# A convolution and SwiGLU kernel: a new order of work for its first three tiles

## Chip, cores and metric

One core of one Trainium2 chip. The metric is device time in microseconds (us), the median of several executions.

## The reference

`x` is [4, 4096, 192], `weight_gen` [4, 4096, 8, 7], `w_gate` and `w_val` [192, 1536], `w_out` [1536, 192].

```python
w = softmax(weight_gen, axis=-1)                # 7 taps per token and head
out = einsum('bshk,bskhg->bshg', w, x_unf)      # causal convolution: token s and the 6 before it
xn = out / sqrt(mean(out * out) + 1e-6) * rms_g
g, val = xn @ w_gate, xn @ w_val
return (silu(g) * val) @ w_out
```

## The kernel before

Each of the 128 partitions holds 128 neighbouring tokens. A tile is four tokens of each partition (`J` = 4, `N` = 512 tokens), so there are 32 tiles, `T` = 0 to 31. Every engine runs its own list of instructions; semaphores written by hand order them.

For a tile, VectorE normalizes the taps (4 steps, `norm_step`) and convolves (13 steps, `conv_step`: 7 products, 6 additions), 17 steps in all. ScalarE squares (`square`), GpSimd makes the inverse root (`inverse_rms`), ScalarE scales (`scale`), TensorE transposes (`turn_x`). ScalarE writes the high part of the transposed tile (`x_high`), VectorE the low part (`x_low`). The up projections have K = 192 as three slots of 64 rows, and gate and value use the two halves of the array side by side; slots 1 and 2 want halves of `xT` on the other partitions, which three DMAs bring (`copy_halves`).

TensorE then makes 12 blocks `f` of 128 hidden columns: `hidden(T, t, f)` is 18 matmuls (w_hi x_hi, w_lo x_hi, w_hi x_lo for three slots and gate and value). ScalarE takes silu, VectorE multiplies (`h`), ScalarE rounds (`h_hi`), VectorE subtracts (`h_lo`), and `project` adds two blocks into `out_ps` with 32 matmuls. `turn_after(T)` is the block after which the next tile is turned: `xf`. `up_ps` has two pairs of banks, so a `hidden` waits for the silu and the product of the block two before it. `out_low` (ScalarE) and `out_add` (VectorE) empty `out_ps` before the next tile's first `project`.

VectorE weaves the 17 steps of tile T + 2 among the blocks of tile T by the list `steps_other`. The first tiles have lists of their own. Tile 0's convolution is made ahead of everything, three tokens of four by VectorE and one by GpSimd; tile 1's by GpSimd alone while tile 0 is multiplied. SyncE issues every DMA. The taps of tiles 3 to 31 get their maxima, differences and exponentials in three pieces (5, 12 and 12 tiles) during tiles 0, 1 and 2; between an exponential and a silu ScalarE loads a function table. TensorE makes 84 transposes of the identity that nobody reads (L699) in the middle of tile 0's convolution.

Of the kernel before, what the change touches and what calls it, by code (L numbers as in the profile page):

```python
# [5 lines left out]
ALU = mybir.AluOpType  # L6
# [7 lines left out]
P = 128  # L14


def dynconv_swiglu(nc, x, weight_gen, w_gate, w_val, w_out, rms_g, out):
# [21 lines left out]
    FIRST = 3  # L39
# [12 lines left out]
    with ExitStack() as ctx:  # L52
# [25 lines left out]
        tap_w1 = sb("tap_w1", [P, J * H, K])  # L78
# [3 lines left out]
        prod_pool = sb("prod_pool", [P, J * D])  # L82
# [31 lines left out]
        x_zeroed = sem("x_zeroed")  # L114
        pool_zeroed = sem("pool_zeroed")
# [19 lines left out]
        x_lo_done = sem("x_lo_done")  # L135
        x_copied = sem("x_copied")
# [25 lines left out]

        cuts = [FIRST, 8, 20, TILES]
        pieces = [slice(a * J * H, b * J * H) for a, b in zip(cuts, cuts[1:])]
# [42 lines left out]
        J0 = J - 1  # L207
        WARM_TURNS = 84
        NORM0_DONE, FIRST_DONE, NORM1_DONE = NORM, MIX, MIX + NORM

        @block.sync
        def _(sp):
# [5 lines left out]

            sp.dma_start(x_first[16:P, 0:PAD, :], x_d[15:P - 1, TOK - PAD:TOK, :]).then_inc(halo_loaded, 16)
            sp.dma_start(x_first[1:16, 0:PAD, :], x_d[0:15, TOK - PAD:TOK, :]).then_inc(halo_loaded, 16)  # L220
            load_taps(0)
            for n in range(2):
                sp.dma_start(x_first[:, PAD + n * J:PAD + (n + 1) * J, :],
                             x_d[:, n * J:(n + 1) * J, :]).then_inc(xfirst_loaded[n], 16)
                if n == 0:
                    load_taps(1)
            sp.dma_start(gains[:, 0:1], g_d[0:P, :]).then_inc(gains_loaded, 16)
            for s in (1, 2):
                for m in range(2):
                    c = CHUNKS[m][s]  # L230
                    sp.dma_start(gains[m * DB:(m + 1) * DB, s:s + 1], g_d[c * DB:(c + 1) * DB, :]).then_inc(gains_loaded, 16)
            for s in range(SLOTS):
                for m, w in enumerate((w_gate, w_val)):
                    c = CHUNKS[m][s]
                    sp.dma_start(raw[m * DB:(m + 1) * DB, s, :], w[c * DB:(c + 1) * DB, :]).then_inc(w_loaded[s], 16)
# [23 lines left out]
            def turn(i, loads=True, first=False, last=False):  # L259
                for t in range(2):  # L260
                    T = 2 * i + t
                    if not (first and t == 0):
                        store(T - 1, (t + 1) % 2)
                    if not (last and t == 1):
# [15 lines left out]
        def _(pool):  # L280
            nc.gpsimd.memset(ident[:], 0.0).then_inc(pool_steps, 1)
            nc.gpsimd.memset(minus_half[:], -0.5).then_inc(pool_steps, 1)
            nc.gpsimd.memset(eps_rms[:], EPS_RMS).then_inc(pool_steps, 1)
            nc.gpsimd.memset(zero[:], 0.0).then_inc(pool_steps, 1)
            pool.wait_ge(pool_steps, 4)
            nc.gpsimd.affine_select(out=ident[:], in_=ident[:], compare_op=ALU.not_equal, fill=1.0, base=0,
                                    pattern=[[-1, P]], channel_multiplier=1).then_inc(consts_done, 1)
# [45 lines left out]
        def _(act):  # L333
# [395 lines left out]
```

## Time and profile before

| | us |
|---|---|
| median of 3 runs | 1323.94 (1322.46 to 1326.7) |
| the profiled execution | 1322.03 |
| its span, first to last instruction | 1320.2 |
| TensorE busy in the span | 1277.4 |
| mean granted TensorE clock | 0.992 |

Times in the trace count from the start of the span; 1.83 us of the profiled execution lie around it. Busy shares are means over the start, the first tiles and the steady tiles, which are read apart below.

### The profile page before, as it was taken

Reading aid. Unit: us, or ns where it says so; the run is one execution under the profiler, and the core shown is the slowest. Engines: PE = TensorE matmul, PEld = TensorE weight load, DVE = VectorE, ACT = ScalarE, POOL = GpSimd, SP = SyncE. Lnnn points to the kernel's source line nnn. Section 1 sums busy time; section 2 is a strip of 40 time slices with the busy share of each in tenths; the row PEclk is TensorE's granted clock in tenths of the full one; section 3 lists DMA queues with packets and bytes.
Section 4 is the critical chain, followed back from the end, with each engine's and each line's share of the span. In section 5 each row is a group of like instructions: output and inputs, shape, how many; then the busy total and the mean of one; then the engine's idle time right before and its main releaser. Section 6 shows DMA issues by size and latency. Waiting matters only on the chain.

```text
span 1320.2 us, 33644 instructions
## 1 busy us (share of the span) xinstructions
PE 1277.4 (97%) x13524; PEld 1260.1 (95%) x13524; DVE 992.0 (75%) x1441; ACT 662.8 (50%) x1427; POOL 83.3 (6%) x101
## 2 busy tenths in 40 slices
PE   3798999999999999999999999999999999999998
PEld 3687889999999999999999999999999999999998
DVE  6788877777777778777778777777777777777653
ACT  4364565445555445555444555444555444555543
POOL 7600000000000000000000000000000000000000
PEclk9799999999999999999999999999999999999999
DMA  9121211211221211221211221111121121121010
GB/s 307 38 67 27 65 58 52 67 56 37 67 67 43 67 55 37 67 67 43 67 55 41 63 67 48 62 55 56 47 67 60 50 67 55 37 67 37 14 37 13
DMA packets 20101, 77.69 MB, mean 59 GB/s; under 512 B 3215, under 2 KB 5007, under 8 KB 19854
## 3 DMA queue, kind: packets, MB, share of 16 engines
q1 hardware_dynamic: 19982, 75.83, 18.9%
q8 instruction: 108, 1.77, 0.5%
q14 instruction: 11, 0.09, 0.0%
HBM read 38.07 MB, written 12.58 MB: 38 GB/s over the span
## 4 chain that ended last, share of the span: by engine, by line
PE 89%; DVE 5%; issue 2%; ACT 2%; DMA 1%; POOL 0%; SPq 0%; POOLq 0%
PE up_ps L620 59%; PE out_ps L651 26%; PE out_ps L655 3%; DVE y L203 1%; DVE h L544 1%; DVE h_lo L562 1%; DMA xT<-xT 1%; DVE prod L201 1%; PE up_ps L588 1%; ACT taps L391 0%; ACT silu L410 0%; PE up_ps L592 0%; DMA taps<-in_weight_gen 0%; ACT h_hi L417 0%; DVE y L201 0%
## 5 line engine op out<-in xcount | busy, mean ns | idle before, releaser
L620 PE MATMUL up_ps<-xT,w_hi 64*128 64x512 f32 x4608 | 858.1, 396 | 14.9 <-DMA xT<-xT 6.5
L620 PEld LDWEIGHTS up_ps<-xT,w_hi 64*128 64x128 f32 x4608 | 627.3, 186 | 26.1 <-issue 8.1
L620 PE MATMUL up_ps<-xT,w_lo 64*128 64x512 f32 x2304 | 589.2, 395 | 0.0
L651 PE MATMUL out_ps<-wo,h_hi 64*128 64x384 f32 x3072 | 478.2, 354 | 3.1 <-issue 2.7
L655 PE MATMUL out_ps<-wo,h_lo 64*128 64x192 f32 x3072 | 453.3, 247 | 0.0
L544 DVE TENSOR_TENSOR h<-up_ps,silu 128x512 f32<-128x512 f32 x384 | 264.7, 689 | 234.1 <-ACT silu L410 233.8
L651 PEld LDWEIGHTS out_ps<-wo,h_hi 64*128 64x128 f32 x3072 | 425.8, 185 | 5.1 <-issue 3.9
L655 PEld LDWEIGHTS out_ps<-wo,h_lo 64*128 64x128 f32 x3072 | 421.2, 187 | 0.5
L417 ACT ACTIVATE h_hi<-h 128x512 fp32r<-128x512 f32 x384 | 242.7, 632 | 352.3 <-DVE h L544 292.0
L410 ACT ACTIVATE silu<-up_ps 128x512 f32<-128x512 f32 x384 | 228.7, 595 | 263.7 <-PE up_ps L620 259.5
L620 PEld LDWEIGHTS up_ps<-xT,w_lo 64*128 64x128 f32 x2304 | 349.5, 187 | 3.3
L562 DVE TENSOR_TENSOR h_lo<-h,h_hi 128x512 fp32r<-128x512 f32 x384 | 265.2, 691 | 40.2 <-ACT h_hi L417 40.2
L203 DVE TENSOR_TENSOR y<-y,prod 128x768 f32<-128x768 f32 (+1 forms) x186 | 177.4, 954 | 2.1
L201 DVE TENSOR_TENSOR prod<-x_buf,tap_w 128x768 f32<-128x768 f32 x180 | 171.1, 951 | 1.5
L292 POOL TENSOR_TENSOR mean_sq<-sq_mean,eps_rms 128x4 f32<-128x4 f32 x32 | 8.2, 258 | 1149.2 <-ACT xn L367 1149.2
L374 ACT ACTIVATE xn<-y,inv_rms 128x128 f32<-128x128 f32 (+1 forms) x256 | 74.1, 360 | 4.4 <-POOL inv_rms L294 4.4
L525 DVE TENSOR_TENSOR last<-out_ps,last 128x768 f32<-128x768 f32 x32 | 30.6, 957 | 27.4 <-ACT last L397 27.4
L367 ACT ACTIVATE xn<-y 128x192 f32<-128x192 f32 x128 | 44.4, 348 | 1.6 <-DVE y L203 1.6
L294 POOL TENSOR_TENSOR inv_rms<-mean_sq,minus_half 128x4 f32<-128x4 f32 x32 | 34.0, 1064 | 2.5
L470 DVE TENSOR_TENSOR xT<-up_ps,xT 128x512 fp32r<-128x512 f32 x32 | 22.1, 691 | 10.7 <-ACT xT L381 9.2
L201 DVE TENSOR_TENSOR y<-x_buf,tap_w 128x768 f32<-128x768 f32 x30 | 28.7, 957 | 1.0
L473 DVE TENSOR_TENSOR xT<-up_ps,xT 64x256 fp32r<-64x256 f32 x64 | 26.6, 416 | 1.0
(43 smaller groups left out, 311.4 us busy)
## 6 DMA issues: line engine op xcount, KB each, us to landing
x_buf<-in_x SPq DMA_DIRECT2D x30, 960.0 KB, 4.5
xT<-xT SPq DMA_DIRECT2D x96, 256.0 KB, 3.8
result<-last SPq DMA_DIRECT2D x32, 384.0 KB, 2.3
taps<-in_weight_gen SPq DMA_DIRECT2D x1, 3248.0 KB, 19.5
raw<-in_moe_w_gate SPq DMA_DIRECT2D x3, 384.0 KB, 6.3
raw<-in_moe_w_val SPq DMA_DIRECT2D x3, 384.0 KB, 7.3
last<-in_moe_w_out SPq DMA_DIRECT2D x1, 1152.0 KB, 12.4
x_first<-in_x SPq DMA_DIRECT2D x2, 384.0 KB, 4.6
```

Source lines behind the costliest of these rows:

```text
L201: return engine.tensor_tensor(heads(product if n else acc), heads(flat(src[:, k + j0:k + j1, :])), w[:, q0:q1, k].unsqueeze(2).to_broadcas ...
L203: return engine.tensor_tensor(acc, acc, product, ALU.add)
L294: nc.gpsimd.tensor_tensor(inv_rms[:], mean_sq[:], minus_half[:], ALU.pow).then_inc(rms_done, 1)
L367: nc.scalar.activation(xn[:, j * D:(j + 1) * D], y[:, t, j, :], ACT.Square, scale=D ** -0.5, accum_out=sq_mean[:, j:j + 1]).then_inc(squar ...
L374: nc.scalar.activation(part[:, j, :], y[:, t, j, d], ACT.Copy, scale=inv_rms[:, j:j + 1]).then_inc(xn_done, 1)
L410: nc.scalar.activation(silu[:, f % 2, :], gate_ps[:, b, :], ACT.Silu).then_inc(silu_done, 1)
L417: nc.scalar.activation(h_hi[:, f % HB, :], h[:, f % 2, :], ACT.Copy).then_inc(h_hi_done, 1)
L544: nc.vector.tensor_tensor(h[:, f % 2, :], val_ps[:, b, :], silu[:, f % 2, :], ALU.mult).then_inc(h_done, 1)
L562: nc.vector.tensor_tensor(h_lo[:, f % HB, :], h[:, f % 2, :], h_hi[:, f % HB, :].bitcast(F32), ALU.subtract).then_inc(h_lo_done, 1)
L620: mm = nc.tensor.matmul(ps[:, banks, :], w[rows, s, cols], xT[rows, t, s, part, :], start=(s == 0 and n == 0), stop=ends)
L651: nc.tensor.matmul(out_ps[:, j, 0:2 * D], h_hi[rows, g % HB, cols], wo[rows, g, :, :].rearrange("p a d -> p (a d)"), start=(g == 0 and k < ...
L655: mm = nc.tensor.matmul(out_ps[:, j, 0:D], h_lo[rows, g % HB, cols], wo[rows, g, 0, :], start=False, stop=(g == FB - 1 and k >= 2), skip_g ...
```

## The change

Start-up: SyncE loads tile 0's taps first; ScalarE issues the gains and the three `w_val` pieces, SyncE the `w_gate` pieces. GpSimd convolves nothing any more. VectorE makes tile 0's seven products over all four tokens into seven tiles, adds the last two, and TensorE sums the six that result with float32 matmuls by the identity (`sum_first`, L704) in `out_ps`, from where they are squared and scaled (half by VectorE, `scale_rest`). There are 50 idle transposes from the start on and 30 after the sum.

Tiles 0 and 1: copies by ScalarE and VectorE inside the engines take the place of `copy_halves` (`x_high_moved`, `x_low_moved`), and the first `hidden` of each takes the matmuls with x_lo last. `w_lo` and `wo` are made in halves. Tile 1 is convolved by VectorE during tile 0, and is squared, scaled and turned only when tile 0's last `project` is through.

From tile 1 on: the lookahead grows from one tile to two by `steps_early`; `turn_after` goes 11, 9, 7, 5. The taps of tiles 4 to 7 are prepared in tile 1, those of later tiles one by one (two in each tile 3 to 14), and their exponentials are taken in tiles 2, 5, 9 and 15. The tile loops of ScalarE and VectorE are written out.

```diff
-    FIRST = 3
+    FIRST = 4
-            return 9 if isinstance(T, int) and T == 0 else 5
+            return {0: 11, 1: 9, 2: 7}.get(T, 5) if isinstance(T, int) else 5
+        exps_at = {(2, 1): (FIRST, 8), (5, 9): (8, 12), (9, 9): (12, 20), (15, 9): (20, TILES)}
-        WARM_TURNS = 84
+        WARM_TURNS, KEEP_TURNS = 50, 30
@@ sync
+            load_taps(0)
 ...
-            load_taps(0)
...
+            load_first(0)
+            load_w(0)
+            load_w(1)
+            load_taps(1)
+            load_w(2)
+            load_first(1)
...
-            copy_halves(0, 0)
@@ scalar
+            first_exps(0)
+            for s in range(SLOTS):
+                act.dma_start(raw[DB:P, s, :], w_val[c * DB:(c + 1) * DB, :]).then_inc(w_loaded[s], 16)
+            w_high(0)
+            w_high(1)
             square(0, 0, range(J))
-            scale(0, 0, range(J))
-            x_high(0, 0, 1)
+            w_high(2)
+            scale(0, 0, range(J // 2))
+            first_exps(1)
+            x_high_moved(0, 0, 1)
@@ scalar, tile
-                squares_at, scales_at = (xf - 4, xf - 3) if first else (0, 1), (xf - 2, xf - 1) if first else (2, 3)
+                squares_at, scales_at = {9: ((6,), (7,)), 7: ((4,), (5, 6)), 5: ((0, 1), (2, 3))}.get(xf, ((), ()))
@@ vector
+            def x_low_moved(T, t, banks):
+                dve.wait_ge(x_hi_done, 3 * T + 1)
+                for to, of in moves(t, 0)[0:2]:
+                    nc.vector.tensor_copy(to, of).then_inc(mid_hi_moved, 1)
+...
+                to, of = moves(t, 1)[2]
+                nc.vector.tensor_copy(to, of).then_inc(end_lo_moved, 1)
-            steps_first = [0, 0, 2, 2, 0, 2, 2, 2, 2, 2, 2, 1]
-            steps_taps = [2, 2, 2, 0, 2, 2, 2, 0, 2, 1, 1, 1]
+            seconds = [0, 0, 1, 1, 2, 2, 2, 1, 2, 2, 0, 0]
+            steps_early = [(2, 4), (2, 2), (2, 2), (2, 2), (2, 2), (2, 2), (2, 3), (3, 0), (3, 0), (3, 0), (3, 4), (3, 2),
...
@@ tensor
+            def sum_first():
+                for k in range(K - 1):
+                    pe.wait_ge(first_mix, NORM + k + 1 if k < K - 2 else FIRST_DONE)
+                    for b in range(2):
+                        cols = slice(b * 2 * D, (b + 1) * 2 * D)
                        mm = nc.tensor.matmul(out_ps[:, b, 0:2 * D], ident[:], first_prods[k][:, cols],
                                              start=(k == 0), stop=(k == K - 2))
...
+                if first:
+                    project(T, FB - 2)
+                    pe.wait_ge(silu_done, xf)
+                    pe.wait_ge(h_done, xf)
+                    pe.wait_ge(xn_done, 4 * J)
+                    turn_x(1, 1, pair(0, xf + 1))
```

TensorE's list at the start. Before:

```order
L699 MATMUL up_ps<-ident 128x128 x84
L588 MATMUL up_ps<-ident,xn 128x64 x8
L592 MATMUL up_ps<-ident,xn 128x64 x4
L620 MATMUL up_ps<-xT,w_hi 128x512 x2
L620 MATMUL up_ps<-xT,w_lo 128x512 x2
L620 MATMUL up_ps<-xT,w_hi 128x512 x4
```

The same place after the change; L862 and L865 are the idle transposes, L715 and L720 the turn, L766 the first `hidden`:

```order
L862 MATMUL up_ps<-ident 128x128 x50
L704 MATMUL out_ps<-prod,ident 128x384 x2
L704 MATMUL out_ps<-y,ident 128x384 x4
L704 MATMUL out_ps<-xn,ident 128x384 x2
L704 MATMUL out_ps<-prod_first,ident 128x384 x2
L704 MATMUL out_ps<-h,ident 128x384 x2
L865 MATMUL up_ps<-ident 128x128 x30
L715 MATMUL up_ps<-ident,xn 128x64 x8
L720 MATMUL out_ps<-ident,xn 128x64 x4
L766 MATMUL up_ps<-xT,w_hi 128x512 x2
```

Twelve matmuls of 384 columns came in, and the idle transposes stand on both sides of them.

VectorE's list from the end of tile 0's tap norm. Before, the first three of 13 steps over 576 columns, each waiting for the one ahead:

```order
L190 TENSOR_TENSOR tap_w<-taps,tap_inv 128x224 [waits first_mix]
L447 TENSOR_REDUCE tap_max<-taps 128x64 [waits first_loaded1,first_mix]
L449 TENSOR_TENSOR taps<-taps,tap_max 128x448 [waits first_steps]
L201 TENSOR_TENSOR y<-x_first,tap_w 128x576 [waits pool_zeroed,x_zeroed,xfirst_loaded0]
L201 TENSOR_TENSOR prod<-x_first,tap_w 128x576 [waits first_mix]
L203 TENSOR_TENSOR y<-y,prod 128x576 [waits first_mix]
```

After the change, in the same place:

```order
L212 TENSOR_TENSOR tap_w<-taps,tap_inv 128x224 [waits first_mix]
L575 TENSOR_TENSOR prod<-x_first,tap_w 128x768 [waits halo_zeroed,halo_loaded,last_zeroed,xfirst_loaded0,first_mix]
L575 TENSOR_TENSOR y<-x_first,tap_w 128x768 x2
L575 TENSOR_TENSOR xn<-x_first,tap_w 128x768
L575 TENSOR_TENSOR prod_first<-x_first,tap_w 128x768
L575 TENSOR_TENSOR h<-x_first,tap_w 128x768
L575 TENSOR_TENSOR silu<-x_first,tap_w 128x768
L578 TENSOR_TENSOR h<-h,silu 128x768 [waits first_mix]
L556 SCALAR_TENSOR_TENSOR w_lo<-raw,gains,w_hi 128x768 [waits w_hi_done] x2
L495 TENSOR_REDUCE tap_max<-taps 128x96 [waits first_loaded1]
```

Thirteen steps became eight, and the other taps' maxima moved behind them.

ScalarE's list in tile 2, where the first late exponential stands (L445 is `out_low`, L458 the silu):

```order
L439 ACT_TABLE_LOAD
L439 ACTIVATE taps<-taps 128x896 [waits rest_less]
L445 ACTIVATE last<-out_ps 128x768 [waits bank_left]
L458 ACT_TABLE_LOAD [waits h_done]
L458 ACTIVATE silu<-up_ps 128x512 [waits gate_done]
```

Before, no exponential stood ahead of an `out_low`; those of the three pieces stood behind block 9.

## Rows read from the trace of the kernel before

**Rows 1.** The page: busy time, share and instructions of each engine.
```profile
PE 1277.4 (97%) x13524; PEld 1260.1 (95%) x13524; DVE 992.0 (75%) x1441; ACT 662.8 (50%) x1427; POOL 83.3 (6%) x101
```

**Rows 2.** Windows: us, busy time and count of each engine, clock, DMA.
```profile
0.00:32.70 32.70, 11.82 (x96) 11.43 (x96) 21.30 (x27) 13.58 (x26) 23.01 (x29) 0.95 0.96 310
32.70:90.70 58.00, 48.26 (x456) 42.54 (x458) 44.33 (x57) 29.04 (x58) 24.02 (x13) 0.88 0.19 53
90.70:212.80 122.10, 114.88 (x1195) 104.44 (x1193) 97.95 (x132) 65.85 (x130) 3.62 (x6) 0.99 0.16 47
212.80:1310.00 1097.20, 1097.20 (x11719) 1096.90 (x11718) 825.35 (x1223) 552.07 (x1212) 32.60 (x54) 1.00 0.18 53
```

**Rows 3.** Timeline: block starts of TensorE, tile 1, then tile 4.
```profile
90.72 0.42 PE L620 MATMUL up_ps<-xT,w_hi 64*128 64x512 f32 x2
...
212.87 0.45 PE L620 MATMUL up_ps<-xT,w_hi 64*128 64x512 f32 x2
...
217.08 0.38 PE L651 MATMUL out_ps<-wo,h_hi 64*128 64x384 f32 x2
...
219.34 0.45 PE L620 MATMUL up_ps<-xT,w_hi 64*128 64x512 f32 x2
```

**Rows 4.** Timeline of the start, all engines: start, duration, instruction, idle before.
```profile
0.74 0.42 SPq L219 DMA_DIRECT2D x_first<-in_x  x1
...
1.73 0.36 SPq L215 DMA_DIRECT2D taps<-in_weight_gen  x1
...
6.61 2.34 ACT L346 ACTIVATE x_first<-zero 1x1152 f32<-1x1152 f32 x2
...
8.19 0.62 DVE L447 TENSOR_REDUCE tap_max<-taps 128x64 f32<-128x448 f32 x1
...
9.39 1.08 DVE L201 TENSOR_TENSOR y<-x_first,tap_w 128x576 f32<-128x576 f32 x1
...
15.73 10.92 PE L699 MATMUL up_ps<-ident 128*128 128x128 f32 x84 [15.73 <-DVE prod L201]
...
19.25 1.58 ACT L352 ACTIVATE w_hi<-raw,gains 128x1536 fp32r<-128x1536 f32 x1 [1.84 <-DMA raw<-in_moe_w_val]
...
22.89 0.36 ACT L367 ACTIVATE xn<-y 128x192 f32<-128x192 f32 x1 [1.60 <-DVE y L203]
...
24.46 1.76 POOL L292 TENSOR_TENSOR mean_sq<-sq_mean,eps_rms 128x4 f32<-128x4 f32 x1 [2.22 <-ACT xn L367]
26.30 2.47 POOL L294 TENSOR_TENSOR inv_rms<-mean_sq,minus_half 128x4 f32<-128x4 f32 x1
```

**Rows 5.** Timeline from the first turn on, all engines.
```profile
31.09 0.69 PE L588 MATMUL up_ps<-ident,xn 64*128 64x64 f32 x8 [4.44 <-ACT xn L374]
...
34.90 1.81 SPq L251 DMA_DIRECT2D xT<-xT  x3
...
40.48 0.80 PE L620 MATMUL up_ps<-xT,w_hi 64*128 64x512 f32 x2 [5.61 <-DMA xT<-xT]
...
43.44 0.60 ACT L410 ACTIVATE silu<-up_ps 128x512 f32<-128x512 f32 x1 [6.82 <-PE up_ps L620]
```

**Rows 6.** Windows of the early drop of the clock; columns as in rows 2.
```profile
29.20:40.40 11.20, 2.92 (x18) 1.54 (x18) 3.68 (x4) 6.38 (x13) 10.73 (x7) 0.50 0.73 256
40.50:46.20 5.70, 5.70 (x28) 4.48 (x30) 2.13 (x2) 1.23 (x2) 5.46 (x4) 0.50 0.01 3
```

**Rows 7.** Groups by line and form: count, busy us, mean ns, idle before.
```profile
L544 DVE TENSOR_TENSOR h<-up_ps,silu 128x512 f32<-128x512 f32 x384 | 264.7, 689 | 234.1 <-ACT silu L410 233.8
...
L203 DVE TENSOR_TENSOR y<-y,prod 128x768 f32<-128x768 f32 x180 | 171.2, 951 | 1.9
...
L473 DVE TENSOR_TENSOR xT<-up_ps,xT 64x256 fp32r<-64x256 f32 x64 | 26.6, 416 | 1.0
...
L391 ACT ACTIVATE taps<-taps 128x2688 f32<-128x2688 f32 x2 | 4.9, 2452 | 0.0
...
L294 POOL TENSOR_TENSOR inv_rms<-mean_sq,minus_half 128x4 f32<-128x4 f32 x32 | 34.0, 1064 | 2.5
```

More of the change, by code:

```diff
@@ L263, in turn @@
                         store(T - 1, (t + 1) % 2)
-                    if not (last and t == 1):
+                    if not (first and t == 0 or last and t == 1):
                         copy_halves(T + 1, 1 - t)
@@ L410, in tile @@
                     nc.scalar.activation(silu[:, f % 2, :], gate_ps[:, b, :], ACT.Silu).then_inc(silu_done, 1)
-                    if f == xf and not last:
+                    if first and f in (0, 4):
+                        wo_high(f // 4)
+                    if f == xf and not (first or last):
                         x_high(T + 1, 1 - t, pair(t, xf + 1))
@@ L609, in hidden @@
                 cols = slice(f * P, (f + 1) * P)
-                for s in range(SLOTS):
-                    if f == 0 and s == 1:
-                        pe.wait_ge(x_copied, 48 * (T + 1))
-                    for n, (w, part) in enumerate(((w_hi, 0), (w_lo, 0), (w_hi, 1))):
-                        if isinstance(T, int) and T == 0 and f == 0:
-                            first_wait(s, n)
-                        ends = s == SLOTS - 1 and n == 2
-                        for m, (ps, done) in enumerate(((gate_ps, gate_done), (val_ps, val_done))):
-                            rows = slice(m * DB, (m + 1) * DB)
-                            mm = nc.tensor.matmul(ps[:, banks, :], w[rows, s, cols], xT[rows, t, s, part, :],
-                                                  start=(s == 0 and n == 0), stop=ends)
-                            if ends:
-                                mm.then_inc(done, 1)
+                parts = ((w_hi, 0), (w_lo, 0), (w_hi, 1))
@@ new lines, in hidden @@
+                steps = [(s, n) for s in range(SLOTS) for n in range(3)]
+                if T < 2 and f == 0:
+                    steps.sort(key=lambda at: at[1] == 2)
+                for at, (s, n) in enumerate(steps):
+                    w, part = parts[n]
+                    if T < 2 and f == 0:
+                        first_wait(T, s, n)
+                    elif f == 0 and s == 1 and n == 0:
+                        pe.wait_ge(x_copied, 48 * (T - 1))
+                    ends = at == len(steps) - 1
+                    for m, (ps, done) in enumerate(((gate_ps, gate_done), (val_ps, val_done))):
+                        rows = slice(m * DB, (m + 1) * DB)
+                        mm = nc.tensor.matmul(ps[:, banks, :], w[rows, s, cols], xT[rows, t, s, part, :],
+                                              start=(at == 0), stop=ends)
+                        if ends:
+                            mm.then_inc(done, 1)
@@ L676, in tile @@
                     if f == 0:
-                        if not first:
+                        if T > 1:
                             project(T - 1, FB - 2)
```

407 lines of the change are left out of this document (256 added, 151 removed).

## The prediction

> **What bounds the kernel now.** I read the page first: TensorE is busy for 97% of the span and VectorE for 75% [rows 1]. That is a mean, so the windows come next. From 212.8 us to 1310 us TensorE is busy in every microsecond, at full clock [rows 2]. A faster VectorE, ScalarE or DMA is worth nothing there, and the change leaves TensorE's work there as it is. All it can win or lose lies ahead of 212.8 us, in three stages: 32.7 us in which TensorE does no useful work, 58 us with 48 busy at a clock of 0.88, and 122 us with 115 busy.
>
> The price of work without waits comes from the block starts of tile 4 [rows 3]: two `hidden` take 217.08 - 212.87 = 4.21 us (2.1 each), two blocks' `project` 2.26, so 6.47 a pair of blocks. Six pairs and a turn (12 transposes, 0.69 us at half clock [rows 5], so some 0.4) make 39.2 us a tile. I measure progress at two marks [rows 3]: A, when tile 0 is projected and tile 1's first two `hidden` are done (90.72), and B, the start of tile 4 (212.87). Between them lie three tiles less one pair, 3 x 39.2 - 6.5 = 111.1 us of work in 122.15, so 11 us are waits.
>
> **The change, part by part.** *To the first sum.* The taps' DMA is issued at 0.74 instead of 1.73, so the tap norm, which ended at 8.19 [rows 4], ends near 7.2. The next maxima (8.19 to 9.39) move out of the way. But the products wait for the zeroing of the halo. ScalarE now issues three DMAs first (an issue is 0.42 on SyncE [rows 4]; I take 0.5 to 0.6) and then zeroes one row, half of 2.34: 6.61 - 1.0 + 1.7 + 1.2 = 8.5. So VectorE stands from 7.2 to 8.5. Seven products and one addition at 0.95 [rows 7] are 7.6 us: 16.1. No row shows a float32 matmul of 384 columns. The nearest row is 84 transposes of the same matrix in 10.92 us [rows 4], 0.13 us per 128 columns, so 0.39. From below the pair of 384 columns within `project` (2.26 us for 16 pairs of 384 or 192 columns, at most 0.2), from above twice the row, 0.78. I take 0.39, whose row has the same operand: a pair, 0.78, hides behind a product of 0.95 and only the last pair shows. Squares start at 16.8 instead of 22.89.
>
> The Trainium skill has a rule against this. *FP8 and Floating Point Precision*, TensorE Precision Notes, says that true float32 takes four passes through the array. By it, 4 x 384 columns at 2.4 GHz are 0.64 us a matmul (an estimate from the page), a pair no longer hides behind its product, and the squares start some 0.6 us later; no row of this trace shows it.
>
> *Sum to turn.* It takes 31.09 - 22.89 = 8.2 us now. GpSimd's two small steps take 1.76 + 2.47 [rows 4] where the power alone is 1.06 on the mean [rows 7]: VectorE was making `w_lo` beside it. VectorE still makes two halves of `w_lo` and the maxima there, so I take 1.9 for the two steps, from 1.4 alone to 4.2. Squares 1.6, scaling halved to 1.2 since VectorE does half. The turn comes at 21.5: 16.8 + 1.6 + 1.9 + 1.2. `w_high(2)` (1.58) stands between squares and scaling, beside GpSimd. It waits for the last weights, whose conversion began at 19.25 [rows 4]; it is free at 18.4 now.
>
> If the two queues work side by side the weights come earlier. The Trainium skill speaks against that: *SBUF — State Buffer*, "Can I just issue two DMAs to hit both halves?", says that two such DMAs serialize on the same 16 engines. By it the third piece would land about as before and the turn move by up to 0.8 us; the row's DMA wait agrees that the weights were late, but shows one queue only.
>
> *Turn to first silu.* Now 43.44 - 31.09 = 12.35 us, 5.6 of them from the DMA issue at 34.90 to 40.48 [rows 5]. The DMA goes. In its place: the exponential of the early taps 0.7, `x_high` main 0.6 (the first row at 22.8), two copies of 64x512 by VectorE, its subtractions 0.69 + 2 x 0.42 [rows 7], the last copy; on ScalarE two rests, one copy, then two after the low part. A copy of 64x512 has no row; 0.42 is the nearest from below (half as long, [rows 7]), 0.69 from above; I take 0.6. The chain is 22.8, 24.0 (copies), 24.7, 25.5, 26.1, plus three pairs of matmuls: gate at 26.5. ScalarE is through at 25.9 and loads the silu table until 27.2. First silu at 27.2, **16.2 us earlier**.
>
> *Tile 0 and mark A.* After that silu 11 `hidden` of tile 0, two of tile 1, six `project` and a turn are 41.3 us of work; now they take 47.3. VectorE's list in tile 0 is 24 products and differences at 0.6 to 0.69, 13 conv steps at 0.95, and three half `w_lo` and two half `wo` (by their length at the conv rate 5 to 6): 34 us beside 38 us of TensorE, with GpSimd's convolution gone from beside it. So tile 0 flows. But tile 1 is no longer turned under cover. The last gate comes at 26.5 + 11 x 2.1 + 4 x 2.26 = 58.6; silu, product, `h_hi` and `h_lo` at 0.6 to 0.69 each, with ScalarE and VectorE just busy, make 61.9, and the last `project` ends at 64.2. ScalarE's squares end at 62.8, rms 64.2, scaling 65.4, turn 65.8, and the chain of copies as above (4.3 us) gives the first gate at 70.1. So TensorE stands for most of 64.2 to 70.1, in which 2.5 us of matmuls fit: a new stall of 3.5. Mark A falls at 72.2 instead of 90.72, **18.5 earlier**.
>
> *Tiles 1 to 3.* The 11 us of waits between A and B do not go; they change place. VectorE has 23 conv and norm steps in tile 1, 26 in tile 2 (22 of them convolutions, 21 us), 19 in tile 3. With 14.5 for 24 block steps (0.69 each alone [rows 7], some 0.6 back to back), 1.5 for `x_low` and 1 for `out_add`, tile 2 holds 39.5 us for a tile of 39.2: VectorE has no slack. Places: tile 1's first `project` waits for `out_add` because four `hidden` follow one another (1.1); in block 6 of tile 1 and 4 of tile 2 ScalarE's squares wait for three conv steps, and the next silu behind them. From the gate on: silu and product 1.3, conv 2.9, squares 1.6, silu and product 1.3, so 7.1, where the second `hidden` after it wants them after 2.1 + 2.26 + 2.1 = 6.5; with VectorE late by 0.6 and 1.2 that is 1.2 and 1.8; the turns wait for the eight scalings just ahead (31.09 less 28.77, 2.3 [rows 4, 5]), 1.5 and 2.4; `rest_subtract` ahead of a product (0.9); tile 2's exponential with two table loads ahead of `out_low` (1). Sum 9.9, and 0.5 of small ones: 10.4 against 11. **0.6 earlier.** The shift of later exponentials, up to 12 tiles' worth (2.45 us [rows 7], and two table loads), falls into steady tiles; only the longest, in tile 15, may overrun the two pairs of banks, **0.5 later**.
>
> *The clock.* Now it is at half, 1.2 GHz, from 29.2 to 46.2 [rows 6]: it fell after the warm transposes ended at 26.65 and rose after work without gap from 40.48. Only the 5.7 busy us from 40.5 cost, 2.9 us. After the change TensorE stands twice: 22 to 26.5, in pieces, and 64 to 70. I expect the clock to fall after either. A return took 5.7 us of full work at half clock, so each costs 0 to 2.9; I take 2 for the second and 1.5 for the first: **3.5 later**.
>
> *Sum*: 16.2 earlier at the silu grows to 18.5 at A, 19.1 at B; less 0.5 and 3.5 it is 15.1, say 15 us. The profiled span of 1320.2 becomes 1305, its execution 1307 (1.8 more). The median of the runs before, 1323.94, is 1.9 above the profiled one; I predict the median: 1323.94 - 15 = **1309 us**.
>
> **Rivals.** *The clock holds and the weave is smooth.* Idle transposes bridge the first gap, the conv steps end before the squares are asked for. Speaks for it: tiles 1 to 3 get a turn later than before, when more is ready. Against: VectorE's 39.5 us in tile 2. It gives back 3.5 and some 3 of the 10.4: 1300 to 1305. Chance 0.17.
>
> *The start is slower than reckoned, or VectorE falls behind.* The upper ends: sums at 0.78 (1.5), GpSimd blocked (2.3), weights late (0.8), clock at its upper bound twice (2.3), stalls in tiles 1 and 2 half as long again (5). Some of these together, 5 to 10 us: 1313 to 1319. For it: each stall above starts from VectorE having no slack. Chance 0.18.
>
> *No change.* The waits only move: TensorE stands as long in tiles 1 and 2 as it gained. It needs 15 us of new waits on top of the 10.4, with VectorE's load at most 39.5 a tile; 1320 to 1328. Chance 0.05.
>
> *Slower.* The tile loops of VectorE and ScalarE are now straight code that must be fetched. A fetch that comes late stalls a silu or a product. VectorE is idle for a quarter of a steady tile [rows 2], 9.7 us; beyond that cover a late fetch shows. It decides at 15 us over 28 steady tiles, 0.54 us of visible stall a tile; at 1 us a tile the time is 1337. Against it: TensorE's 13524 matmuls [rows 1] are straight code already and show no gap after 212.8. Chance 0.05.
>
> **Numbers.** My forecast has 0.55, with its own range 1305 to 1313. The range of 1302 to 1316 leaves out the faster end of the first rival, the far end of the second, and the last two: 2 in 10. Faster by over 0.3% (about what a measurement of this kernel can tell from no change) 0.90, within it 0.05, slower 0.05.
>
> **What would show it.** Right: squares near 17, turn near 21.5, first silu near 27, marks A and B near 74 and 197, TensorE without a gap afterwards, two drops of the clock, near 25 and 67. Wrong: the sum's matmuls over 0.7 us each; GpSimd's power over 2 us; the first product later than 9; gaps of TensorE after mark B; a third stretch at half clock.

## The result, and the profile after

The changed kernel takes 1299.21 us (median of 4 runs, 1298.18 to 1300.5) where the kernel before took 1323.2 (1322.24 to 1326.7, now four runs): a ratio of 0.9816 with an interval of 0.9801 to 0.9831, 24 us faster where 15 were forecast, and outside the range. The profiled execution took 1299.58 with a span of 1297.4, so the spans differ by 22.8. Line numbers have moved in the changed kernel: L766 is `hidden`, L806 and L810 `project`, L715 and L720 the turn, L704 the sum, L649 `h`, L458 the silu.

The page of the changed kernel, its busy times (compare [rows 1]) and its row of the clock over the slices: TensorE does as much, 4 us less of busy time, and its clock shows no slice below 9 tenths.

```profile
PE 1273.1 (98%) x13544; PEld 1240.3 (96%) x13544; DVE 1001.0 (77%) x1511; ACT 663.9 (51%) x1428; POOL 42.8 (3%) x76
...
PEclk9999999999999999999999999999999999999999
```

The windows up to the first `hidden`, up to mark A, up to mark B and behind it; columns as in [rows 2]. The first stage is 9 us shorter, the clock is 1.00 in every stage, and behind B there are 3.4 us without TensorE where there were none.

```profile
0.00:23.70 23.70, 19.65 (x116) 15.84 (x117) 14.77 (x24) 11.12 (x21) 5.12 (x14) 1.00 0.92 246
23.70:73.10 49.40, 45.42 (x458) 40.54 (x460) 41.10 (x66) 26.48 (x52) 1.21 (x2) 1.00 0.23 97
73.10:195.00 121.90, 113.42 (x1196) 103.07 (x1193) 105.06 (x154) 60.65 (x133) 3.96 (x6) 1.00 0.19 55
195.00:1293.00 1098.00, 1094.62 (x11784) 1080.81 (x11780) 839.07 (x1269) 564.99 (x1224) 32.53 (x54) 1.00 0.18 53
```

The timeline of the start, all engines (compare [rows 4]). The first product comes at 8.89; the sum's matmuls of one product fill 1.3 us (13.88, 15.17, 16.46; a float32 matmul leaves two records, so x4 is a pair); squares at 18.13, the turn at 22.33, the first silu at 27.82.

```profile
8.89 0.96 DVE L575 TENSOR_TENSOR prod<-x_first,tap_w 128x768 f32<-128x768 f32 x1 [2.07 <-DMA x_first<-in_x]
...
13.88 1.45 PE L704 MATMUL out_ps<-xn,ident 128*128 128x384 f32 x4
...
15.17 1.45 PE L704 MATMUL out_ps<-prod_first,ident 128*128 128x384 f32 x4
...
16.46 1.45 PE L704 MATMUL out_ps<-h,ident 128*128 128x384 f32 x4
...
18.13 0.31 ACT L392 ACTIVATE xn<-out_ps 128x192 f32<-128x192 f32 x1
...
19.55 0.20 POOL L328 TENSOR_TENSOR mean_sq<-sq_mean,eps_rms 128x4 f32<-128x4 f32 x1 [11.03 <-ACT xn L392]
19.78 1.58 ACT L372 ACTIVATE w_hi<-raw,gains 128x1536 fp32r<-128x1536 f32 x1 [0.32 <-DMA raw<-in_moe_w_val]
19.82 1.02 POOL L330 TENSOR_TENSOR inv_rms<-mean_sq,minus_half 128x4 f32<-128x4 f32 x1
...
22.33 0.46 PE L715 MATMUL up_ps<-ident,xn 64*128 64x64 f32 x8 [1.14 <-ACT xn L400]
...
23.59 0.88 DVE L528 CAST xT<-xT 64x512 fp32r<-64x512 f32 x2 [0.79 <-ACT xT L412]
...
27.82 0.60 ACT L458 ACTIVATE silu<-up_ps 128x512 f32<-128x512 f32 x1
```

TensorE's block starts in tile 4 (compare [rows 3]), then the starts of tiles 17 and 28.

```profile
194.95 0.44 PE L766 MATMUL up_ps<-xT,w_hi 64*128 64x512 f32 x2
...
199.10 0.36 PE L806 MATMUL out_ps<-wo,h_hi 64*128 64x384 f32 x2
...
201.38 0.44 PE L766 MATMUL up_ps<-xT,w_hi 64*128 64x512 f32 x2
...
705.47 0.48 PE L766 MATMUL up_ps<-xT,w_hi 64*128 64x512 f32 x2
...
1134.07 0.47 PE L766 MATMUL up_ps<-xT,w_hi 64*128 64x512 f32 x2
```

The same starts of tiles 17 and 28 in the kernel before:

```profile
723.50 0.41 PE L620 MATMUL up_ps<-xT,w_hi 64*128 64x512 f32 x1
...
1155.61 0.41 PE L620 MATMUL up_ps<-xT,w_hi 64*128 64x512 f32 x1
```

These are eleven tiles with no wait in either. From start to start, one took before the change (1155.61 - 723.50) / 11 = 39.28 us; now (1134.07 - 705.47) / 11 = 38.96. The instructions are the same. The `hidden` pair shows it (199.10 - 194.95 = 4.15, where [rows 3] have 4.21) and `project` does not (2.28 against 2.26).

So the gain of the span is: first silu 15.6 earlier (43.44 to 27.82); mark A 17.7 (90.72 to 73.06); mark B 17.9 (212.87 to 194.95); behind B, 28 tiles of 0.32 less make 8.9, and new waits in tiles 6 to 16 take back 4.0. 17.9 + 8.9 - 4.0 = 22.8. (The profiled executions differ by 22.45, because 2.2 us instead of 1.8 lie around the span. The medians differ by 24.0: that of before lies 1.2 above its profiled execution, that of the changed kernel 0.4 below.) The prediction had no term for the 8.9.

### The profile page after: what moved, and what is told of

It reads as the page before. It is cut to its first block, busy times and chain, and to the rows that moved or that the text cites. A ratio compares the mean times of both kernels' runs of the same rounds, so it can differ in the third digit from the quotient of the medians.

```text
span 1297.4 us, 32473 instructions
## 1 busy us (share of the span) xinstructions
PE 1273.1 (98%) x13544; PEld 1240.3 (96%) x13544; DVE 1001.0 (77%) x1511; ACT 663.9 (51%) x1428; POOL 42.8 (3%) x76
## 4 chain that ended last, share of the span: by engine, by line
PE 86%; DVE 6%; ACT 3%; issue 3%; DMA 1%; ACTq 0%; POOL 0%; DVEq 0%
PE up_ps L766 55%; PE out_ps L806 21%; PE out_ps L810 9%; DVE h L649 2%; DVE y L225 1%; DMA raw<-in_moe_w_val 1%; DVE prod L223 1%; DVE h_lo L675 1%; ACT silu L458 1%; PE up_ps L715 1%; ACT L458 0%; ACT xn L400 0%; ACT L439 0%; ACT xn L392 0%; PE up_ps L720 0%
## 5 line engine op out<-in xcount | busy, mean ns | idle before, releaser
L766 PE MATMUL up_ps<-xT,w_hi 64*128 64x512 f32 x4608 | 816.2, 392 | 8.5 <-DVE h L649 5.4
L766 PEld LDWEIGHTS up_ps<-xT,w_hi 64*128 64x128 f32 x4608 | 527.2, 184 | 25.9 <-issue 8.6
L766 PE MATMUL up_ps<-xT,w_lo 64*128 64x512 f32 x2304 | 502.5, 387 | 0.0
L806 PE MATMUL out_ps<-wo,h_hi 64*128 64x384 f32 x3072 | 465.0, 356 | 7.1 <-issue 2.4
L810 PE MATMUL out_ps<-wo,h_lo 64*128 64x192 f32 x3072 | 437.2, 247 | 0.0
L649 DVE TENSOR_TENSOR h<-up_ps,silu 128x512 f32<-128x512 f32 x384 | 264.6, 689 | 209.0 <-ACT silu L458 205.9
L806 PEld LDWEIGHTS out_ps<-wo,h_hi 64*128 64x128 f32 x3072 | 357.5, 184 | 11.2 <-issue 3.3
L810 PEld LDWEIGHTS out_ps<-wo,h_lo 64*128 64x128 f32 x3072 | 362.4, 187 | 0.9
L458 ACT ACTIVATE silu<-up_ps 128x512 f32<-128x512 f32 x384 | 227.9, 594 | 246.0 <-PE up_ps L766 237.5
L766 PEld LDWEIGHTS up_ps<-xT,w_lo 64*128 64x128 f32 x2304 | 269.2, 185 | 6.3
L225 DVE TENSOR_TENSOR y<-y,prod 128x768 f32<-128x768 f32 x186 | 177.3, 953 | 2.1
L400 ACT ACTIVATE xn<-y,inv_rms 128x128 f32<-128x128 f32 x244 | 70.6, 360 | 1.4 <-POOL inv_rms L330 1.4
L445 ACT ACTIVATE last<-out_ps 128x768 f32<-128x768 f32 x32 | 25.3, 790 | 3.7 <-PE out_ps L810 3.7
## 6 DMA issues: line engine op xcount, KB each, us to landing
last<-in_moe_w_out SPq DMA_DIRECT2D x1, 1152.0 KB, 18.1
x_first<-in_x SPq DMA_DIRECT2D x2, 384.0 KB, 10.8
```

The lines of the kernel that those rows point to most:

```text
L225: return engine.tensor_tensor(acc, acc, product, ALU.add)
L400: nc.scalar.activation(part[:, j, :], src, ACT.Copy, scale=inv_rms[:, j:j + 1]).then_inc(xn_done, 1)
L458: nc.scalar.activation(silu[:, f % 2, :], gate_ps[:, b, :], ACT.Silu).then_inc(silu_done, 1)
L649: nc.vector.tensor_tensor(h[:, f % 2, :], val_ps[:, b, :], silu[:, f % 2, :], ALU.mult).then_inc(h_done, 1)
L766: mm = nc.tensor.matmul(ps[:, banks, :], w[rows, s, cols], xT[rows, t, s, part, :], start=(at == 0), stop=ends)
L806: nc.tensor.matmul(out_ps[:, j, 0:2 * D], h_hi[rows, g % HB, cols], wo[rows, g, :, :].rearrange("p a d -> p (a d)"), start=(g == 0 and k < ...
```

## The experiments

**Where do 0.32 us a tile come from?** The change also removes the tile `tap_w1` (224 floats, 896 bytes of each partition), in which GpSimd kept tile 1's taps, so everything declared behind it, `xT` among it, lies 896 bytes lower. Theory A: the addresses set the pitch of the `hidden` matmuls, the time from one start to the next. Its rival: the new order of work does. `x1_pad` gives the changed kernel a tile that nobody uses and that puts `xT` where it was; `x2_shift` gives the kernel before the new addresses.

```diff
# x1_pad, on the changed kernel
         tap_w = sb("tap_w", [P, J * H, K])
+        spare = sb("spare", [P, J * H, K])
# x2_shift, on the kernel before: the declaration moves to the end
-        tap_w1 = sb("tap_w1", [P, J * H, K])
...
+        tap_w1 = sb("tap_w1", [P, J * H, K])
```

> The changed kernel with one unused tensor of 896 bytes a partition put back where the removed tap_w1 stood, so that every tensor declared behind it has the address it had before the change. A steady tile takes 38.96 us in the changed kernel and 39.28 us in the one before, though TensorE has the same list there. Theory A (where xT, w and h lie in SBUF sets the pitch of the matmul pairs): a steady tile returns to 39.28 us and the time rises by 27 x 0.32 = 8 to 9 us, to about 1308 us. Theory B (the pitch comes from something else in the change, such as the written-out loops or the clock): a steady tile stays at 38.96 and the time at about 1299 us.

> The kernel before with tap_w1 declared last, so that the tensors behind it move down by 896 bytes a partition; nothing else changes. Theory A: a steady tile takes 38.96 us instead of 39.28 and the time falls by 9 to 10 us, to about 1314 us. Theory B: no change, 1323 us.

`x1_pad` took 1308.76 (1307.33 to 1310.02), a ratio to before of 0.9894 (0.9877 to 0.991): the new order of work alone is worth 13.8 us against the 1322.55 of the same chip. (Its four executions are 1307.33, 1307.5 and twice 1310.02, with a mean granted clock of 1.000, 1.000 and twice 0.996, so the 13.8 is good to some 1.3 us.) `x2_shift` took 1314.75 (1314.71 to 1315.21), 0.9937 (0.9921 to 0.9954): the kernel before gains 7.8 us from a declaration that moves. Starts of tiles 17 and 28 of `x1_pad`:

```profile
709.00 0.45 PE L767 MATMUL up_ps<-xT,w_hi 64*128 64x512 f32 x2
...
1141.08 0.45 PE L767 MATMUL up_ps<-xT,w_hi 64*128 64x512 f32 x2
```

And of `x2_shift`:

```profile
720.84 0.46 PE L620 MATMUL up_ps<-xT,w_hi 64*128 64x512 f32 x2
...
1149.44 0.45 PE L620 MATMUL up_ps<-xT,w_hi 64*128 64x512 f32 x2
```

(1141.08 - 709.00) / 11 = 39.28 us a tile in the changed kernel, (1149.44 - 720.84) / 11 = 38.96 in the kernel before: the tile goes with the addresses in both. The order of work as the cause fell; theory A stands. `x1_pad` starts tile 4 at 194.70, so ahead of mark B the addresses gained nothing. `x2_shift` gained less than 28 x 0.32 = 9 us: its profiled execution reaches mark B 1.45 us later than before (214.32 against 212.87), with one more drop of the clock in tile 0.

**Do the idle transposes keep the clock up?** `x3_nokeep` takes away the 30 behind the sum.

```diff
-        WARM_TURNS, KEEP_TURNS = 50, 30
+        WARM_TURNS, KEEP_TURNS = 50, 0
```

> The changed kernel without the 30 idle transposes after the sum; TensorE then stands in one piece from 17.8 us to 22.3 us. Theory C (the idle transposes are what kept the clock up over the first gap, as the prediction's first rival had it): the granted clock falls to half near 22 us and returns within some 6 us of work; the first silu is later and the time 1 to 4 us longer. Theory D (the clock would have held anyway): no stretch at half, and the time as it is, 1299 us.

It took 1301.45 (1299.54 to 1301.82), 2.2 more than the changed kernel, but its profiled execution of 1299.54 equals that of the changed kernel, 1299.58. Windows of it around the two short drops of the clock that this execution shows:

```profile
22.70:26.10 3.40, 2.78 (x13) 2.14 (x14) 2.73 (x7) 2.98 (x6) 0.00 (x0) 0.54 1.02 413
26.10:67.00 40.90, 38.43 (x410) 35.84 (x406) 34.56 (x50) 20.42 (x42) 1.21 (x2) 1.00 0.22 92
67.00:70.40 3.40, 3.23 (x16) 2.26 (x18) 2.71 (x6) 2.55 (x6) 0.00 (x0) 0.55 0.00 0
```

Both drops lie where TensorE stands in pieces anyway: by the starts of the turns, tile 0 is no longer for them and tile 1 by 0.4 us. The drops that theory C expects are there, but the transposes don't decide them: `x4_exps7`, below, keeps all 30, and its execution has the clock at half for 3.4 us three times, from 23.8, 68.2 and 139.9 on. Nor does the program alone decide. `x_best` and `x_split_p192`, further down, are the same kernel, and in the same stretch the execution of `x_best` shows half clock:

```profile
67.10:70.50 3.40, 3.40 (x17) 2.40 (x16) 2.16 (x5) 1.94 (x4) 0.00 (x0) 0.51 0.00 0
```

and that of `x_split_p192` full clock:

```profile
67.10:70.50 3.40, 2.75 (x18) 1.61 (x20) 2.58 (x6) 2.38 (x5) 0.00 (x0) 1.00 0.00 0
```

From the turn of tile 1 to that of tile 2 the first takes 35.83 us and the second 35.32: this drop costs 0.5. What the 30 transposes are worth stays open: the medians differ by 2.2 us, the ranges overlap (1299.54 to 1301.82 and 1298.18 to 1300.5), and executions of one kernel with the transposes differ by as much (1307.5 and 1310.02 in `x1_pad`).

**The late exponentials.** Those of tiles 5, 9 and 15 stand behind block 9 in the changed kernel. `x4_exps7` moves them to block 7.

```diff
-        exps_at = {(2, 1): (FIRST, 8), (5, 9): (8, 12), (9, 9): (12, 20), (15, 9): (20, TILES)}
+        exps_at = {(2, 1): (FIRST, 8), (5, 7): (8, 12), (9, 7): (12, 20), (15, 7): (20, TILES)}
```

> The changed kernel with the three late exponentials moved from block 9 to block 7 of tiles 5, 9 and 15. After block 9 two convolution steps stand between the product of block 10 and that of block 11; after block 7 the same pair has two and one, so only the DVE work right behind differs little. Theory E (the stalls of 0.6, 1.35 and 2.1 us in those tiles come from VectorE's convolution steps behind the late silu): with block 7 the stalls stay about as they are or shrink by under 1 us in all. Theory F (they come from rest_subtract and the turn of the tile, which other blocks do not have): they shrink by more than 2 us, time 1296 to 1297 us.

It took 1297.22 (1296.04 to 1298.67), 0.9801 (0.9784 to 0.9817); two of its four executions show a mean clock of 0.999 and take 1296.1, two show 0.996 and 0.997 and take 1298.5. In the changed kernel they lengthen tiles 6, 9, 10, 15 and 16 by 0.57, 0.30, 1.05, 1.04 and 1.05 us by the tile starts, 4.0 in all; here 1.8 are left, in tiles 9 and 15. So 2.3 went, and theory E's "under 1 us" is wrong. F's number came, but its reason did not: in the rows of tile 5 below, `rest_subtract` (268.08 to 268.47) is over long before VectorE's late product, and the turn lies blocks earlier. What moved is told with those rows. `x_split` also cuts the exponentials to the length of four tiles each.

```diff
-        exps_at = {(2, 1): (FIRST, 8), (5, 9): (8, 12), (9, 9): (12, 20), (15, 9): (20, TILES)}
+        exps_at = {(2, 1): (FIRST, 8), (5, 7): (8, 12), (9, 7): (12, 16), (11, 7): (16, 20),
+                   (15, 7): (20, 24), (17, 7): (24, 28), (19, 7): (28, TILES)}
```

> The changed kernel with its late exponentials in six pieces of four tiles, behind block 7 of tiles 5, 9, 11, 15, 17 and 19, instead of pieces of 4, 8 and 12 tiles behind block 9. In the run with block 7, the piece of four tiles cost no stall, the one of eight 0.66 us and the one of twelve 1.1 us. Theory G (a stall begins only where table loads and exponential together outlast the cover, so what counts is the length of each piece): all stalls go, 4.0 us less than the changed kernel, about 1295 us, and every tile from 4 on takes 38.96 us. Theory H (each pair of table loads has a price of its own): six pieces cost as much as three, 1297 us or more.

It took 1295.23 (1294.72 to 1295.47), 0.9784 (0.9768 to 0.98), 4.0 less than the changed kernel. A window behind mark B of the changed kernel:

```profile
195.00:1280.00 1085.00, 1082.35 (x11646) 1069.00 (x11644) 833.99 (x1262) 560.48 (x1216) 32.53 (x54) 1.00 0.19 54
```

The same window of `x_split`: TensorE is busy in every microsecond.

```profile
195.00:1280.00 1085.00, 1085.00 (x11690) 1030.27 (x11688) 836.30 (x1264) 570.46 (x1228) 32.65 (x54) 1.00 0.19 54
```

**Which property of the address?** The next runs put a tile of a few floats ahead of `xT`. By the addresses that the tiles were given, in the changed kernel `w_hi`, `w_lo` and `wo` lie 160 bytes behind a multiple of 256 in each partition, `xT` 224; in the kernel before `xT` lies 96 behind. `h_hi` and `h_lo` follow `xT`, so what is said of `xT` and the weights holds for `h_hi` and `wo` too.

```diff
# x_p32: 8 floats; x_p128, x_p256, x_p384: 32, 64, 96; x_split_p160, _p192, _p224: 40, 48, 56 on x_split
+        spare = sb("spare", [P, 8])
         xT = sb("xT", [P, 2, SLOTS, 2, N], F32R)
```

> The changed kernel with 32 unused bytes a partition ahead of xT, so that xT, silu, h, h_hi and h_lo begin at a multiple of 512 bytes. The nine slots of a hidden block then read xT rows that begin at a multiple of 512. Theory A1 (what counts is how the matmul's moving rows lie against a boundary of 64 to 512 bytes): the pitch of a pair of blocks differs from 6.43 us, probably below it, and with it the tile from 38.96 us. Theory A2 (only a coarse distance between the tensors counts): the tile stays at 38.96 us.

> The same with 128 bytes. Theory A1: the tile differs from 38.96 us. Theory A2: 38.96 or 39.28 us.

> The same with 256 bytes. Theory A1: another pitch than with 128 bytes, if the period is 512; the same as with 0 bytes, 38.96 us, if it is 256 or less. Theory A2: 38.96 or 39.28 us.

> The same with 384 bytes, which is 896 less 512. If the effect has a period of 512 bytes this gives the tile of 39.28 us that 896 bytes give; if its period is longer, another one.

> The same with 160 unused bytes ahead of xT: xT begins 128 bytes behind a multiple of 256. So far 224 behind gives tiles of 38.96 us (twice), 96 gives 39.28 to 39.29 (four times), 0 gives 39.36. Theory A1 (the place within 256 bytes sets the pitch): a value of its own between 38.9 and 39.4 us. Theory A3 (a distance to w_hi and w_lo, which begin 160 behind, sets it: 64 apart is fast, 96 and 192 apart slow): 224 apart, a value of its own too.

> The same with 192 bytes: xT begins 160 bytes behind a multiple of 256, as w_hi, w_lo and wo do. Theory A3 makes this an extreme, fastest or slowest; theory A1 puts it between its neighbours.

> The same with 224 bytes: xT begins 192 bytes behind a multiple of 256. Theory A1 puts it near the 224 of the changed kernel, 38.96 us.

A shift by 256 bytes brings the pitch back, 128 and 384 give the same slow one, and a shift of 192 bytes gives one that neither kernel had, 38.63 us a tile, with `xT` and the weights both 160 behind a multiple of 256. That left two readings: A1, the place of `xT` by itself (160 is good), and A3, its distance to the weights. `x_both224` and `x_both0`, both made from `x_split`, move `w_hi` and all behind it too, so that both lie 224, and both 0, behind.

```diff
# x_both224, on x_split; x_both0 has 24 floats for the first
+        spare_w = sb("spare_w", [P, 16])
         w_hi = sb("w_hi", [P, SLOTS, F], F32R)
...
+        spare = sb("spare", [P, 48])
         xT = sb("xT", [P, 2, SLOTS, 2, N], F32R)
```

> The kernel with six pieces, with 64 unused bytes ahead of w_hi and 192 ahead of xT: w_hi, w_lo, wo, xT, h_hi and h_lo all begin 224 bytes behind a multiple of 256. xT has the very address of the run with 256 bytes, whose steady tile took 38.96 us; only the weights have moved by 64. Theory A3 (the distance between the weights and xT, modulo 256, sets the pitch): 38.63 us, as when both were at 160; a time near 1285 us. Theory A1 (the place of xT alone sets it): 38.96 us, 1295 us.

> The same with 96 and 192 bytes: all of them begin at a multiple of 256. Theory A3: 38.63 us. Theory A1: 39.36 us, as in the run with 32 bytes, whose xT began at a multiple of 256. If both the place and the distance count, something else, perhaps below 38.63.

Both have 38.63. `x_both224` has `xT` at the very address of `x_p256`, where a tile took 38.96, so the address of `xT` alone is not it, and A3 stands. The distance to VectorE's tiles is not it either: from `xn` to `xT` it is the same in the kernel before and in `x2_shift`, 39.28 and 38.96. All kernels by the distance from the weights to `xT`, modulo 256 bytes; the tile is a steady one without waits. The kernels of this group (`x_p...`, `x_split_p...`, `x_both...`) were executed once each, and their times also hold between none and three early drops of the clock, so the pitch is what counts:

| distance | kernels (us) | tile, us |
|---|---|---|
| 0 | `x_split_p192` 1285.43, `x_both224` 1285.27, `x_both0` 1287.79, `x_before160` 1305.91 | 38.63 to 38.64 |
| 32 | `x_split_p224` 1306.45 | 39.28 |
| 64 | changed kernel 1299.21, `x_p256` 1301.43, `x_split` 1295.23, `x2_shift` 1314.75 | 38.96 |
| 96 | `x_p32` 1311.11 | 39.36 |
| 192 | before 1323.2, `x1_pad` 1308.76, `x_p128` 1307.94, `x_p384` 1308.69 | 39.28 to 39.29 |
| 224 | `x_split_p160` 1305.65 | 39.32 |

**Does it hold for the kernel before, and what is the best of both?** `x_before160` is the kernel before with 16 floats ahead of `xT` (distance 0); `x_best` is `x_split_p192` once more, executed four times.

```diff
# x_before160, on the kernel before
+        spare = sb("spare", [P, 16])
         xT = sb("xT", [P, 2, SLOTS, 2, N], F32R)
```

> The kernel before with 64 unused bytes ahead of xT, so that xT begins 160 bytes behind a multiple of 256 as its weights do; nothing else changes. Theory A3: a tile of 38.63 instead of 39.28 us, 30 tiles x 0.65 = about 19 us less, near 1304 us. If the effect belongs to the new order of work, nothing: 1323 us.

> The kernel of x_split_p192 again, timed: the new first tiles, the exponentials in six pieces, and xT at the same place modulo 256 as the weights. One look gave 1285.4 us; I expect 1285.5 us, 1.1% below the changed kernel and 2.9% below the one before, ratio to the kernel before 0.971.

`x_before160` took 1305.91 (1303.29 to 1306.78), 0.9871 (0.9855 to 0.9888); `x_best` 1285.14 (1285.12 to 1287.05), 0.9717 (0.97 to 0.9734). Tile starts of `x_best`, 4, then 17 and 28, with the first `project` pair of tile 4:

```profile
194.05 0.49 PE L768 MATMUL up_ps<-xT,w_hi 64*128 64x512 f32 x2
...
198.17 0.41 PE L808 MATMUL out_ps<-wo,h_hi 64*128 64x384 f32 x2
...
200.42 0.49 PE L768 MATMUL up_ps<-xT,w_hi 64*128 64x512 f32 x2
...
696.40 0.43 PE L768 MATMUL up_ps<-xT,w_hi 64*128 64x512 f32 x2
...
1121.36 0.43 PE L768 MATMUL up_ps<-xT,w_hi 64*128 64x512 f32 x2
```

(1121.36 - 696.40) / 11 = 38.63. The `hidden` pair takes 4.12, `project` 2.25. The group of L620 by form, in the kernel before:

```profile
L620 PE MATMUL up_ps<-xT,w_hi 64*128 64x512 f32 x4608 | 858.1, 396 | 14.9 <-DMA xT<-xT 6.5 <-DVE h L544 6.0 <-DVE xT L473 1.6
```

The same group of `x_best`. The mean of one matmul, 396 and 390 ns, shows little of it: matmuls overlap, and what changes is the distance between their starts.

```profile
L768 PE MATMUL up_ps<-xT,w_hi 64*128 64x512 f32 x4608 | 792.2, 390 | 5.4 <-DVE h L651 3.0 <-ACT xT L414 1.6 <-ACT xT L423 0.5
```

With the distance held at 192, the new order of work is worth 13.8 us (`x1_pad`); with it held at 0, the new order and the split exponentials are worth 1305.91 - 1285.14 = 20.8. The profiled executions give 1303.29 - 1285.16 = 18.1, which is near 13.8 and the 4.0 of the exponentials together. The other executions of `x_before160` are 1.9 to 3.5 us longer at the same mean clock (0.991); no trace of them shows why.

## Why the prediction was wrong

**The step that failed** is in the first paragraph: that the change "leaves TensorE's work there as it is". It leaves the instructions, and moves the operands. The steady tile was taken at 39.2 and as the same on both sides; it measured 39.28 before and 38.96 after, 8.9 us over 28 tiles, shown by `x1_pad` and `x2_shift` in both directions. Without it the changed kernel is `x1_pad`, 13.8 us faster than before, beside the 15 forecast, and its 1308.76 would have been the 1309 of the forecast. That is partly luck, because terms cancel: 1.2 less was gained up to mark B, the exponentials cost 3.5 more, and the clock 3.5 less. Of the five signs of being wrong that the prediction names one came, gaps behind mark B; the pitch was not among them.

**To the first sum: right in its chain, short in two terms.** The first product was put at 8.5 and came at 8.89, but not for the zeroing that the step blamed, whose last part ended at 8.52 on GpSimd: the row names the DMA of `x_first`, which landed at 8.81 and so 2.5 us later than before (6.26), with taps, gains and weights issued beside it. The sum's pair was taken at 0.78, hidden behind a product of 0.95; it takes 1.29. So TensorE, not VectorE, sets the end of the sum, and the squares start at 18.13 instead of 16.8. The Trainium skill (*FP8 and Floating Point Precision*, TensorE Precision Notes: true float32 takes four passes) led to the estimate of 0.64 a matmul; the trace agrees, with 1.29 / 2 = 0.645. The row of the transposes was the wrong neighbour.

**Sum to turn.** GpSimd's two steps took 1.3 (19.55 to 20.84), not 1.9, with no `w_lo` of VectorE beside them, and gave back part of it: the turn is at 22.33 against 21.5. The third weight piece was converted at 19.78, where [rows 4] have 19.25: two queues brought it no earlier. That is what the Trainium skill says of two such DMAs (*SBUF — State Buffer*, "Can I just issue two DMAs to hit both halves?"), and the trace agrees: the piece landed at 19.76, before the change at 19.23. It cost 0.4 us of the 0.8 that the prediction allowed for: GpSimd is through at 20.84 and VectorE begins its half of the scaling at 20.88, but ScalarE, busy with the conversion until then, begins its half at 21.27, and the turn waits for ScalarE.

**Turn to silu.** 5.5 us against 5.7 forecast; a copy of 64x512 takes 0.44, not 0.6. The silu came 15.6 us earlier, 16.2 forecast.

**Marks A and B.** The new stall before tile 1 was right in kind and place: the last `project` ends near 65.4 (64.2 forecast), the turn is at 66.19 (65.8), tile 1's first silu at 71.19. The rows of that stretch, all engines:

```profile
65.15 0.25 PE L810 MATMUL out_ps<-wo,h_lo 64*128 64x192 f32 x2
...
66.19 0.46 PE L715 MATMUL up_ps<-ident,xn 64*128 64x64 f32 x8 [0.79 <-ACT xn L400]
...
67.56 0.50 PE L766 MATMUL up_ps<-xT,w_hi 64*128 64x512 f32 x2 [0.78 <-ACT xT L412]
...
70.42 0.97 PE L766 MATMUL up_ps<-xT,w_hi 64*128 64x512 f32 x6 [0.56 <-ACT xT L421]
...
71.19 0.60 ACT L458 ACTIVATE silu<-up_ps 128x512 f32<-128x512 f32 x1 [0.82 <-PE up_ps L766]
```

Mark A is at 73.1 (72.2 forecast ahead of the clock), B 17.9 earlier (19.1). Waits between them are 10.8 us at the prediction's price of work (121.9 less 111.1), 10.4 forecast, and 11.4 at the new pitch: they changed place and did not go.

**The clock: wrong by 3.5.** It was forecast at half after both gaps, at 1.5 and 2 us. In the profiled execution of the changed kernel it stays at 2.4 GHz through both. Where another execution shows the drop before tile 1, it costs 0.5 (`x_best` beside `x_split_p192`), and the one of `x3_nokeep` at the start costs nothing that tile 0's length shows. Executions of `x1_pad` and `x4_exps7` that differ in their mean clock by 0.002 to 0.004 differ in time by about 2.5 us, so in some executions of these kernels the clock does take that much. Behind the last `project` of tile 0 TensorE never stands for 1 us at a stretch (0.79, 0.78 and 0.56 in the rows above), because the first `hidden` takes what is ready; before the change it stood 5.61 us [rows 5]. That this is why a drop is short is argued, not shown: no run varied the length of the gap, and one kernel has the drop in one execution and not in the other.

**Late exponentials: right in kind, too small.** 0.5 forecast, only in tile 15; 4.0 measured, in three places. The rows of tile 5, all engines:

```profile
267.38 1.28 ACT L439 ACT_TABLE_LOAD   x1
...
268.68 0.95 ACT L439 ACTIVATE taps<-taps 128x896 f32<-128x896 f32 x1
...
269.65 1.28 ACT L458 ACT_TABLE_LOAD   x1
...
270.94 0.60 ACT L458 ACTIVATE silu<-up_ps 128x512 f32<-128x512 f32 x1
...
271.57 0.69 DVE L649 TENSOR_TENSOR h<-up_ps,silu 128x512 f32<-128x512 f32 x1 [3.10 <-ACT silu L458]
...
272.18 0.95 DVE L225 TENSOR_TENSOR y<-y,prod 128x768 f32<-128x768 f32 x1
...
273.16 0.96 DVE L223 TENSOR_TENSOR prod<-x_buf,tap_w 128x768 f32<-128x768 f32 x1
...
274.04 0.68 DVE L675 TENSOR_TENSOR h_lo<-h,h_hi 128x512 fp32r<-128x512 f32 x1
274.64 0.68 DVE L649 TENSOR_TENSOR h<-up_ps,silu 128x512 f32<-128x512 f32 x1
...
275.47 0.51 PE L766 MATMUL up_ps<-xT,w_hi 64*128 64x512 f32 x2 [0.32 <-DVE h L649]
```

The silu is late by two table loads and an exponential of four tiles, and TensorE does not stand for that. But VectorE, late with one product, then makes its two convolution steps and `h_lo` before the next product (272.18 to 274.64), and the `hidden` after that waits. The prediction priced the exponential and forgot what is queued behind the late instruction on VectorE.

That queue is not the whole of it. `x4_exps7` has the same queue behind its late product in tile 5, and no stall:

```profile
261.75 1.28 ACT L439 ACT_TABLE_LOAD   x1
...
265.94 0.69 DVE L649 TENSOR_TENSOR h<-up_ps,silu 128x512 f32<-128x512 f32 x1 [3.11 <-ACT silu L458]
...
269.01 0.68 DVE L649 TENSOR_TENSOR h<-up_ps,silu 128x512 f32<-128x512 f32 x1
```

From product to product it takes the same 3.07 us (274.64 - 271.57 and 269.01 - 265.94). What differs is the start: in the changed kernel the first table load begins 0.93 us after TensorE begins the block that the late silu belongs to (267.38 and 266.45), in `x4_exps7` 0.25 us after (261.75 and 261.50). By the rows of VectorE, ScalarE is late there because two convolution steps stand ahead of block 9's product and only one ahead of block 7's. The tile is 0.57 us longer; a start 0.7 us earlier is enough. So the stall is a sum: what VectorE does ahead of the exponential, the two loads and the exponential, and what is queued behind. With the exponentials two blocks earlier and none over four tiles it is gone (`x_split`).

**The rivals.** The first, smooth weave and full clock, put the time at 1300 to 1305; the clock did hold, but the waits of the weave stayed at 11.4, so its number was nearly met for another reason. Of the second, only the slower sum came, and its upper bound of 0.78 a pair was too low. Late code fetch did not show: from 195 to 1280 `x_split` has no gap.

## What to carry to other kernels

Before timing a change of schedule, compare the addresses of every operand of the bounding engine's instructions, and hold them where they were; a tile that is removed or declared elsewhere is a change of its own, here worth 8 to 18 us. Where a stall is priced, count what stands ahead of the late instruction and behind it on its engine, until the next one that the bounding engine waits for. Do not read the clock from one execution: the same kernel can show a drop in one and none in another. And read the pitch from start to start over many tiles: a steady tile that differs by 0.3 us is as good as a stage.

## What was unexpected of the hardware

In this kernel the pitch of the matmuls that use the two halves of the array side by side depends on the distance between the moving operand (`xT`) and the weights in a partition, modulo 256 bytes. A steady tile of 216 `hidden` and 192 `project` matmuls takes 38.63 us at distance 0, 38.96 at 64 and 39.28 to 39.36 at 32, 96, 192 and 224. Most of it is in `hidden`: by the starts in tile 4, a pair of blocks is 4.21, 4.15 and 4.12 us at distances 192, 64 and 0, and six pairs of 0.09 are 0.54 of the 0.65. `project` hardly moves: 2.26, 2.28 and 2.25 us in the same tile. Open are why, what lies between the six distances tried, and whether `wo` and `h_hi`, whose distance changed along in every run, have a part; no run moved one pair without the other. The identity and the taps lie behind the weights and moved with them, but in these blocks TensorE reads neither.
